# Attention of two units at a time, pairs of heads outermost, and one more weight unit beside it

## The reference

```python
# 1: attention, 2 sequences x 8 heads x 768 positions x 64
scores = q @ k.T / sqrt(64)
keep = (column < 8) | ((row - column >= 0) & (row - column < 96))
scores = where(keep, scores - slope[head] * distance, -1e9)
a = softmax(scores); attn = a @ v                # -> x, 1536 x 512
# 2: soft mixture: 32 slots, 4 for each of 8 experts
logits = x @ phi; d = softmax(logits, over tokens); c = softmax(logits, over slots)
slot_out[e] = relu((d.T @ x)[e] @ w1[e]) @ w2[e]
x = c @ slot_out
# 3: sparse mixture: each token goes to the 2 best of 8 experts
out[token] += weight * (relu(x[token] @ w1[e]) @ w2[e])
```

## Time and profile before

| | |
|---|---|
| median of 3 runs | 392.98 us (391.38 to 393.2) |
| the profiled execution: its own time | 392.51 us |
| the profiled execution: its span | 389.8 us |
| TensorE, VectorE, ScalarE, GpSimd busy | 93%, 49%, 44%, 55% |
| transfers | 88.85 MB, mean 228 GB/s |
| attention, first matmul to the last heads | about 10 to 108 us |
| dispatch and layer 2 | about 108 to 162 us |
| layer 3 | about 162 to 377 us |

### The profile page before, as it was taken

The page is one execution under the profiler, slowest core; times in us unless marked ns, Lnnn a source line. Parts: engine busy times, 40 slices in busy tenths (PEclk is TensorE's granted clock), DMA queues, the critical chain, the costliest instruction groups (busy, mean ns, idle before and its releaser), DMA issues.

```text
span 389.8 us, 8657 instructions
## 1 busy us (share of the span) xinstructions
PE 362.6 (93%) x2892; PEld 251.6 (65%) x2892; DVE 192.7 (49%) x639; ACT 170.4 (44%) x429; POOL 213.3 (55%) x422
## 2 busy tenths in 40 slices
PE   6899999999997999589799999999999999999990
PEld 5566666666564443256577777777777777777770
DVE  2699988888853011068172452623525426254210
ACT  2566777776541110043273453524525336253310
POOL 3568866667811040011446777747766576766741
PEclk9699999999999999889899999999999999999996
DMA  7987999999799999998577899876869762332432
GB/s 161 238 243 224 222 268 298 279 258 374 278 401 347 401 398 387 398 405 330 174 268 170 249 269 250 236 170 145 267 145 209 224 139 34 43 47 32 57 43 38
DMA packets 71976, 88.85 MB, mean 228 GB/s; under 512 B 41616, under 2 KB 42112, under 8 KB 71936
## 3 DMA queue, kind: packets, MB, share of 16 engines
q1 hardware_dynamic: 66448, 79.84, 62.7%
q0 software_dynamic: 5200, 8.49, 15.4%
q10 hardware_dynamic: 288, 0.00, 0.0%
HBM read 77.33 MB, written 10.99 MB: 227 GB/s over the span
## 4 chain that ended last, share of the span: by engine, by line
PE 59%; DVE 16%; issue 15%; DMA 8%; ACT 1%; DVEq 1%; POOL 0%; POOLq 0%; ACTq 0%
PE y_bank L1574 26%; PE y_bank L1577 13%; DMA weight_ring<-in_moe_w 6%; PE h_banks L1563 5%; DVE arena L1031 4%; DVE row_sum L1039 4%; PE bank L1509 3%; PE bank L1261 2%; PE y_bank L1478 2%; DVE row_inv L1053 2%; PE h_banks L1446 2%; PE h_banks L1261 1%; DVE arena L933 1%; DVE arena L1047 1%; DMA counts_i<-in_n_local 1%
## 5 line engine op out<-in xcount | busy, mean ns | idle before, releaser
L1213 DVE SCALAR_TENSOR_TENSOR hT_lo<-h_banks,hT_hi 128x512 fp32r<-128x512 f32 x56 | 38.5, 689 | 110.3 <-ACT hT_hi L866 104.8
L1574 PE MATMUL y_bank<-w_hi,hT_hi 128*128 128x512 f32 x224 | 91.6, 409 | 0.8 <-ACT hT_hi L866 0.8
L1574 PE MATMUL y_bank<-w_lo,hT_hi 128*128 128x512 f32 x224 | 88.2, 394 | 0.0
L866 ACT ACTIVATE hT_hi<-h_banks 128x512 fp32r<-128x512 f32 x56 | 33.4, 597 | 98.8 <-PE y_bank L1577 51.8
L610 POOL TENSOR_TENSOR arena<-arena,row_inv 128x512 f32<-128x512 f32 (+1 forms) x48 | 49.5, 1032 | 29.2 <-DVE row_inv L1053 27.1
L547 POOL TENSOR_TENSOR turn_mark<-turn_mark 128x1 f32<-128x1 f32 x135 | 41.4, 310 | 38.1 <-DMA out_rows<-arena,add_row 12.6
L1577 PE MATMUL y_bank<-w_hi,hT_lo 128*128 128x512 f32 x224 | 59.9, 389 | 0.0
L782 ACT ACTIVATE arena<-arena,neg_max 128x256 f32<-128x256 f32 (+1 forms) x96 | 46.3, 483 | 26.8 <-DVE neg_max L1031 25.8
L705 POOL DMA_INDIRECT out_rows<-arena,add_row x28 | 44.8, 1599 | 14.1 <-issue 13.0
L1574 PEld LDWEIGHTS y_bank<-w_hi,hT_hi 128*128 128x128 f32 x224 | 44.2, 197 | 11.2 <-issue 3.0
L1574 PEld LDWEIGHTS y_bank<-w_lo,hT_hi 128*128 128x128 f32 x224 | 42.8, 191 | 7.9
(11 more groups left out here) (196 smaller groups left out, 494.6 us busy)
## 6 DMA issues: line engine op xcount, KB each, us to landing
weight_ring<-in_moe_w SPq DMA_DIRECT2D x16, 2048.0 KB, 13.2
weight_ring<-in_moe_w SPq DMA_DIRECT2D x22, 1024.0 KB, 5.5
arena<-in_moe_w SPq DMA_DIRECT2D x5, 2048.0 KB, 12.1
arena<-in_q SPq DMA_DIRECT2D x16, 192.0 KB, 5.8
arena<-in_k SPq DMA_DIRECT2D x16, 192.0 KB, 5.4
arena<-in_v SPq DMA_DIRECT2D x8, 384.0 KB, 4.8
out_rows<-zero_row SPq DMA_DIRECT2D x2, 1536.0 KB, 10.4
out_rows<-arena,add_row POOLq DMA_INDIRECT x28
```

The lines of the kernel that those rows point to most:

```text
L1213: vec.scalar_tensor_tensor(hidden_of(hT_lo, half), h_banks[half][:, :, 0:FR], 0.0, hidden_of(hT_hi, half), ALU.max, ALU.subtract).then_inc ...
L1574: mm(y_of(i), hT_hi[:, n, :], w[e % 2][:, n, :], start=(n == 0 and w is w_hi), stop=False)
```

## The change

- TensorE, VectorE and ScalarE run over groups of two units, 24 of them. Group s has the scores of units 2s and 2s+1; head h of both units shares one bank (`score_cols`), so the scores of a group wait until all four logits of the group before are read, and VectorE starts a group only when all its scores are there.
- TensorE's turn is now: the transposes of the probabilities of two units (group s-2), four transposes of q and k (in every group up to the last pair, into banks 0 and 3 in turn, which lets them run one store further ahead), the scores of group s, the heads of group s-2.
- VectorE's turn: four logits, then twice the sum, the reciprocal, and the copy of a unit of group s-1. The sums are of the same group as the logits, and no copy lies between sum and reciprocal any more.
- ScalarE's turn: the store of q and k, the store of heads, then four exponentials.
- Pairs of heads are outermost, so pairs 0, 2, 4 and 6 start new heads: two biases are made in each of pairs 0, 2 and 4, into `bias4`, from operands kept in columns of xT.
- Three transposes of x are issued ahead of the last group's transposes of probabilities; only the fourth one remains behind the product with phi.
- Seven units have a place beside attention and are issued after pairs -1 to 5; no zero rows are. After 42 heads SyncE issues unit 7 and then both halves of the zero rows (3 MB), and after all heads units 8 and 9.

The general path (other counts than those given) is adapted and isn't run here. The rest of the diff moves views of memory.

```diff
-    EARLY = 6
-    DURING = 4
+    EARLY = 7
+    DURING = 3
...
-        v_own[0], v_win[0], qT[0], kT[0] = view(2, QB, HD), view(2, QB - 2, HD), view(S), view(QB, WIN)
-
-        bias8 = view(H, BCOLS)
...
+        for s in range(2):
+            v_own[s], qT[s], kT[s] = view(2, QB, HD), view(S), view(QB, WIN)
+        GENERAL_AT = top[0]
+        v_win = [view(2, QB - 2, HD) for _ in range(2)]
+        bias4 = view(4, BCOLS)
         prob = [view(2, WIN) for _ in range(4)]
         probT = [view(2, 2, P) for _ in range(2)]
...
-        v_win[1], v_own[1], qT[1], kT[1] = view(2, QB - 2, HD), view(2, QB, HD), view(S), view(QB, WIN)
...
-        rel, col, penalty = [view(BCOLS) for _ in range(3)]
+        rel, col = [view(BCOLS) for _ in range(2)]
+        rel_kept, penalty = [xT[:, 0:BCOLS // P, hp, :] for hp in (PAIRS - 1, PAIRS - 2)]
...
-        def score_bank(u, h):
-
-            return bank[1 + (2 * u + h) % 3]
+        GROUPS = UPB * B // 2
+        def score_cols(u, h):
...
+            return bank[1 + h][:, u % 2 * WIN + (P if u % QB == 0 else 0):(u % 2 + 1) * WIN]
+        def qk_bank(n):
+            return bank[3 * (n % 2)]
...
-        ZERO_AFTER = (PAIRS - 1, NPAIR - 4)
+        ZERO_PARTS = 2
...
             def load_v(p):
-                b, hp = divmod(p, PAIRS)
+                hp, b = divmod(p, B)
...
-                if p in UNIT_AFTER:
-                    load_unit(UNIT_AFTER.index(p))
...
-
-                    sp.wait_ge(zeros_made, 1)
-                    part = ZERO_AFTER.index(p)
-                    first, end = [TT * n // len(ZERO_AFTER) for n in (part, part + 1)]
-                    sp.dma_start(out.rearrange("(n p) d -> p n d", p=P)[:, first:end, :],
-                                 zero_row[:].unsqueeze(1).to_broadcast([P, end - first, DM])).then_inc(rows_zeroed, 16)
+                load_unit(p + 1)
...
-                if n == EARLY + 2:
+                if n == EARLY + 1:
+                    sp.wait_ge(zeros_made, 1)
+                    for part in range(ZERO_PARTS):
...
+                        sp.dma_start(out.rearrange("(n p) d -> p n d", p=P)[:, rows, :],
+                                     zero_row[:].unsqueeze(1).to_broadcast([P, TT // ZERO_PARTS, DM])).then_inc(rows_zeroed, 16)
...
                     sp.wait_ge(heads_ready, UPB * B)
...
+                def next_pair(s):
+                    n = s + 3
+                    if n < 3 * NPAIR:
+                        store_qk(n // 3 % 2, n % 3, n, qk_bank(n))
+                for s in range(GROUPS + 3):
+                    if 0 < s < GROUPS:
+                        next_pair(s)
+                    for w in (2 * s - 6, 2 * s - 5):
+                        if w >= 0 and w % HALF == HALF - 1:
+                            store_heads(w // HALF, w + 1)
+                    if s < GROUPS:
+                        for u in (2 * s, 2 * s + 1):
+                            off = P if u % QB == 0 else 0
+                            for h in range(2):
+                                act.wait_ge(logits_ready, 2 * u + h + 1)
+                                own = prob[u % 4][:, h, off:]
+                                last = nc.scalar.activation(own, own, ACT.Exp, bias=neg_max[:, u % 2, h:h + 1], scale=-1.0,
+                                                            accum_out=row_sum[:, u % 4, h:h + 1])
+                            last.then_inc(exps_ready, 1)
+                    if s == 0:
+                        next_pair(s)
...
+                vec.scalar_tensor_tensor(by_block(bias4[:, h % 4, :]), rel_kept, -SLOPES[h] / SCALE, penalty, ALU.mult, ALU.add).then_inc(bias_made, 1)
...
+                    dve.wait_ge(exps_ready, u + 1)
+                    vec.tensor_scalar(row_sum[:, u % 4, :], row_sum[:, u % 4, :], EPS, None, ALU.add).then_inc(sums_ready, 1)
+                    dve.wait_ge(sums_ready, u + 1)
+                    vec.reciprocal(row_inv[:, u % 4, :], row_sum[:, u % 4, :]).then_inc(inv_ready, 1)
+                def store_probT(u):
...
+                for s in range(GROUPS + 1):
+                    p, j = divmod(s, 3)
+                    if s < GROUPS:
+                        if j == 0 and p % B == 0:
+                            dve.wait_ge(bias_made, 2 * (p // B + 1))
+                        dve.wait_ge(scores_ready, s + 1)
+                        if s >= 2:
+                            dve.wait_ge(probT_ready, 2 * s - 2)
...
-                        dve.wait_ge(sums_ready, w + 1)
-                        vec.reciprocal(row_inv[:, w % 4, :], row_sum[:, w % 4, :]).then_inc(inv_ready, 1)
-                    if p < PAIRS - 1 and i in (2, 4):
-                        make_bias(2 * (p + 1) + i // 2 - 1)
+                        for k in range(2):
+                            logits(2 * s + k)
+                    for k in range(2):
+                        if s < GROUPS:
+                            sums(2 * s + k)
+                        if s >= 1:
+                            store_probT(2 * s - 2 + k)
+                    if j and p % B == 0 and p // B + 1 < PAIRS:
+                        make_bias(2 * (p // B + 1) + j - 1)
...
+            def first_x():
+                pe.wait_ge(out_bank_free, HALVES * B)
+                for t in range(3):
+                    transpose_x(t)
...
+                def scores(s):
+                    p, j = divmod(s, 3)
+                    if j == 0:
...
+                        pe.wait_ge(window_ready, 2 * p + 1)
...
+                        pe.wait_ge(window_ready, 2 * p + 2)
+                    if s >= 1:
...
+                        pe.wait_ge(logits_ready, 4 * s)
+                    for u in (2 * s, 2 * s + 1):
...
+                            last = mm(score_cols(u, h), qT[p % 2][own, i * P:(i + 1) * P],
+                                      kT[p % 2][own, i, off:], start=True, stop=True)
                     last.then_inc(scores_ready, 1)
...
+                def transpose_next(s):
+                    n = s + 3
+                    if n < 3 * NPAIR:
+                        p, j = divmod(n, 3)
+                        if j == 0:
+                            pe.wait_ge(qk_loaded[p % 2], QK_DMAS * (p // 2 + 1))
+                        pe.wait_ge(qk_stored, n - 1)
+                        transpose_qk(p % 2, j, n, qk_bank(n))
...
+                for s in range(GROUPS + 2):
+                    if s == GROUPS + 1:
+                        pe.wait_ge(logits_ready, 4 * GROUPS)
+                        first_x()
+                    if s >= 2:
+                        for u in (2 * s - 4, 2 * s - 3):
+                            transpose_probs(u)
+                    if 0 < s < GROUPS:
+                        transpose_next(s)
+                    if s < GROUPS:
+                        scores(s)
+                    if s == 0:
+                        transpose_next(s)
+                    if s >= 2:
+                        for u in (2 * s - 4, 2 * s - 3):
+                            heads(u)
...
-            for t in range(2, 4):
-                transpose_x(t)
+            transpose_x(3)
```

More of the change, by code:

```diff
@@ L469, in _ @@
             load_v(1)
-            UNIT_AFTER = [p for p in range(-1, NPAIR - 2) if p != PAIRS - 1]
-            assert len(UNIT_AFTER) == EARLY
+            assert NPAIR - 1 == EARLY
             for p in range(-1, NPAIR - 2):
@@ L746, in store_heads @@
             def store_heads(hv, done):
[L748 to L749 removed]
+                p, half = divmod(hv, QB // HALF)
+                hp, b = divmod(p, B)
+                token = S * b + half * HALF * P
                 act.wait_ge(heads_ready, done)
[L751 removed]
+                copy(xT[:, token // P:token // P + HALF, hp, :],
                      bank[6 + hv % 2][:, 0:HALF * P].rearrange("p (t n) -> p t n", n=P)).then_inc(out_bank_free, 1)
@@ new lines, in logits @@
+                def logits(u):
+                    hp = u // QB // B
+                    n0, nb = bias_cols(u % QB)
+                    for h in range(2):
+                        vec.tensor_tensor_reduce(
+                            out=prob[u % 4][:, h, WIN - nb:], in0=score_cols(u, h),
+                            in1=bias4[:, hp % 2 * 2 + h, n0:n0 + nb], scale=-SCALE, scalar=3.0e38,
+                            op0=ALU.add, op1=ALU.min, accum_out=neg_max[:, u % 2, h:h + 1]).then_inc(logits_ready, 1)
@@ L1273, in transpose_qk, with transpose_x @@
                 last.then_inc(qk_transposed, 1)
+            def transpose_x(t):
+                if t >= 4:
+                    pe.wait_ge(x_stored_vec if t % 2 else x_stored_act, (t - 4) // 2 + 1)
+                for c in range(DC):
+                    last = transpose(bank[t % 4][:, c * P:(c + 1) * P], xT[:, t, c, :])
+                last.then_inc(x_ready, 1)
+            def first_x():
+                pe.wait_ge(out_bank_free, HALVES * B)
+                for t in range(3):
+                    transpose_x(t)
             pe.wait_ge(consts_made, 1)
```

125 lines of the change are left out of this document (27 added, 98 removed).

## The result

The changed kernel takes 394.5 us (median of 18 executions, 392.4 to 403.4), the kernel before, on the same chip, 391.7 (387.8 to 399.4, 18 executions). The ratio is 1.0083, 95% interval 1.0054 to 1.0112: slower by 0.8%, 3.3 us. Ratios compare only executions outside a slower state that either kernel now and then falls into (up to 403 us here), so they can differ a little from the ratio of the medians. The range of the prediction (388 to 398) holds the median; its likeliest case, no change within 0.5%, did not happen.

The account below looks back on a forecast made before the run. TensorE was taken to bound attention, then transfers released by `part_ready`; VectorE would become attention's bound. `part_ready` 0.3 later takes the profiled 392.5 to 392.8; the median, 0.5 above, gives 393.2, range 388.0 to 398.0.

Parts of the forecast that it names:

- The three rivals in attention: Attention: sum ahead of product, 389.0, nearly all of 0.33; TensorE kinds stay dear, 395.7, 0.17; whole GpSimd hold, 400, 0.05.
- the fourth, by transfers: Transfers: zero rows at two thirds of the rate end the backlog at 126.7, 1.5 longer; chance 0.06.
- no change: Whole kernel: time within 0.5%, 2 us, for itself 391.3 to 395.2; chance 0.39.
- 395.7: Rival in attention: TensorE's kinds stay as dear as now, group 4.05, pair 11.5, 2 more and 0.5; chance 0.17.
- Each bias now costs its whole 0.80 less an overlap of 0.07.: VectorE without slack in attention: six biases in pairs 0, 2 and 4 make these 12.5.
- Pair without bias 11.0: VectorE in attention: groups of 3.2, 3.8 and 4.0 make 11.0 a pair, more than TensorE's 10.8.
- The first logits stay at 11.66: Start of attention: first two biases and first load of q and k as before, so no shift.
- The last pair: End of attention: last heads about 108.75, product with phi at 109.3, 0.3 later than before.
- The 42nd heads at 97.1, the backlog through 2 us ahead of unit 10.: SyncE's transfers: heads 2.4 earlier; 9.4 MB at 404 GB/s end at 122.5 or 123.1, unit 10's first bytes at 125.2.
- the end moves with `part_ready`: Layer 2's transfers: unit 15 lands 36.3 behind `part_ready`, if transfers issued before it are through by then.
- TensorE 3.8 a group: TensorE in attention: 3.8 a group against about 4.0 before, 10.8 a pair, 0.8 less.
- the first rival: Attention: second sum slips ahead of GpSimd's product, TensorE holds the pairs at 10.8, 4.2 less, 389.0; nearly all of 0.33.

Follow-up runs that it names:

- experiments 3: Changed kernel without the additions of 1e-9 to the sums of exponentials: 386.7 us, ratio 0.9851 to the kernel before.
- experiment 4: Changed kernel with two more transposes of probabilities a group on TensorE: ratio 1.0032 to the kernel before.
- 7: Kernel before without the additions of 1e-9 to the sums of exponentials: ratio 0.9972.
- experiment 1: Changed kernel without the six biases VectorE makes inside attention, later heads reusing those of heads 0 and 1: ratio 0.9974 to the kernel before.
- experiment 2: Changed kernel with the two operands of the biases in one contiguous piece of the weight ring's last slot: ratio 1.0057 to the kernel before.
- experiment 5: Changed kernel with both additions to the sums kept, the group's second sum moved behind both copies: 388.9 us, ratio 0.9912 to the kernel before.
- 8: Changed kernel without the additions to the sums, SyncE issuing q and k ahead of the weight unit: 388.3 us, ratio 0.9846 to the kernel before.
- 9: Changed kernel with its twelve first transposes of x back behind the last heads: ratio 1.0078 to the kernel before.
- 11: Changed kernel without additions to the sums, q and k ahead of weight units, biases inside attention by ScalarE: 383.4 us, ratio 0.9785 to the kernel before.
- 12: Changed kernel with ScalarE's biases, q and k ahead of weight units, both additions kept, the second behind both copies: 388.4 us, ratio 0.9867.
- experiment 10: Changed kernel with three useless matrix products ahead of the first scores and four behind them: 395.4 us, ratio 1.0107 to the kernel before.

## What the prediction had right and wrong, step by step

The picture held: VectorE became the bound (experiments 3 and 4 against 7), the second sum is held to the end of GpSimd's product, and nothing is won by what TensorE spares. The three rivals in attention did not happen; the fourth, by transfers, did in part. The sizes missed by 1.7 us at `part_ready`, forecast at 122.8 and measured at 124.5, and the chance of 0.39 for "no change" went with them. That 394.5 nevertheless lies within the 391.3 to 395.2 given for that case is luck: the forecast started from a median of 392.98, and the kernel before then measured 391.7. Of the rivals, 395.7 is the nearest number, but experiment 4 excludes its mechanism.

- **"Each bias now costs its whole 0.80 less an overlap of 0.07."** This is the term that failed. Beside GpSimd a bias takes 0.93 or 1.28 (47.21 above), because it waits for GpSimd's operation and then takes its own 0.67 (rows in the last section). Pairs 2 and 4 took 13.16 and 13.18 where 12.5 was forecast. The pair behind pair 2 gave 0.34 back, so its two biases cost 1.65, those of pair 4 about 2.0; forecast was 1.5. All six held up pair 7 by about 5.4 (experiment 1) where 4.5 was forecast: 0.9 of the 1.7. I had priced them by the row 45.11 0.80, and had looked for GpSimd's hold at the sums alone.
- **Pair without bias 11.0**: 10.84 in pairs 1 and 3, 11.20 and 11.19 in pairs 5 and 6. Groups 3.12 or 3.46, 3.83, 3.90 against 3.2, 3.8, 4.0. Right in size; experiment 1, without biases, has 11.18. The sum of all distances came out 1.26 over the forecast, +1.34 from pairs 2 and 4, +0.39 from pairs 5 and 6, -0.47 from the other three.
- **"The first logits stay at 11.66"**: 12.07, because the operands moved into columns of xT (11.54 with contiguous operands, experiment 2). It cost nothing by itself, since the second group starts at 14.6 with or without it.
- **The last pair**: 16.18 where 16.1 was forecast, 15.68 before.
- **The 42nd heads at 97.1, the backlog through 2 us ahead of unit 10.** They came at 98.9, and by the forecast's own 2 + 23.4 the backlog would end at 124.3, 2.6 ahead of unit 10's first bytes (124.5 + 2.4). Yet no gap was left, which I had named as a sign of being wrong. So the rate failed too. In the stretch in which zero rows were written it was not 375 or 404 (windows of the changed kernel):

```profile
104.00:106.00 2.00, 0.83 (x12) 0.65 (x14) 1.63 (x4) 0.80 (x3) 1.70 (x2) 1.00 0.87 238
106.00:108.00 2.00, 2.00 (x23) 1.83 (x21) 0.00 (x0) 0.00 (x0) 2.00 (x8) 1.00 0.92 324
```

  That is about 1.2 us of transfers lost against 404. From 98 to 124 us 8.8 MB moved (339 GB/s), so of the backlog of 9.4 MB 0.6 MB were left, and it ended near 125.6 or later (an estimate from these rates). The fourth rival's rate, two thirds, came true for these 4 us; its 1.5 at the end did not. In the changed kernel the price is small: unit 15 lands 36.6 behind `part_ready`, not 36.3. But where `part_ready` follows the issue of unit 7 more closely, the backlog and no longer `part_ready` sets the end: with 24.5 to 25.2 us between the two (experiments 3, 5, 8, 9, 11 and 12) unit 15 lands 37.0 to 37.7 behind `part_ready`, with 25.7 (the changed kernel, 2, 4 and 10) 36.1 to 36.6; experiment 1, a slower execution, has 25.7 and 37.2. So "the end moves with `part_ready`" held only just. The 358 GB/s weighed in that step (the Trainium skill, SBUF — State Buffer, Summary: rules for kernel authors) are passed here too, with 418 and 390 in the first two windows above: the trace disagrees with that page again.
- **TensorE 3.8 a group**: about 3.5, from rows with no wait (experiment 4). Heads take 1.03 for two units and not 1.18, scores 1.06 and not 1.12. I had taken distances in a kernel in which each kind stood alone. This did not change the sum, but it made the first rival worth 4.2 in the text; when experiment 5 took most of the hold away, 5.0 came at pair 7 and 6.7 in time.

Of the 3.3 us measured, 2.35 are followed from rows. The other 0.9 is not followed. It is less than single profiles differ by from the last expert on, and the drop of the clock at the start can have a part in it; how often that drop comes to either kernel stays open. The two profiles compared here differ in it: the kernel before was granted 0.50 from 12 to 18 us, the changed one 1.00. What the drop costs the old order is not known, since all three profiles of it have one.

## What to carry to other kernels

When an engine becomes the bound, price its instructions by what they take beside the other engines in the new order, not by the shortest row of the old one; small operations and long ones are held differently. Look for the instruction that waits in the middle of such a chain and move it, before taking work away: the order of two small sums was worth about as much as all six biases (6.7 us of time against 4.3; 5.0 at pair 7 against about 5.4). When a backlog is to be hidden behind a later event, follow it by the bytes that moved and not by the best rate. And when a step speeds one engine, list who gives slack back and who is late next (here q and k behind a 2 MB unit).

## What was not expected of the hardware

- A `tensor_scalar` of 128x2 on VectorE is held by GpSimd's product (0.53 in place of 0.17), a `reciprocal` of 128x2 is not (0.17 in the midst of one), nor are the copies from PSUM (0.69 throughout). The bias, which reads two arrays from SBUF, is held, and holds GpSimd in turn. Pair 2 of the changed kernel, VectorE and then GpSimd:

```profile
42.54 0.93 DVE L948 SCALAR_TENSOR_TENSOR arena<-arena 128x640 f32<-128x640 f32 x1
```

```profile
42.29 0.51 POOL L586 COPY arena<-arena 128x384 f32<-128x384 f32 x1
42.76 1.61 POOL L613 TENSOR_TENSOR arena<-arena,row_inv 128x512 f32<-128x512 f32 x1
...
46.77 1.04 POOL L613 TENSOR_TENSOR arena<-arena,row_inv 128x512 f32<-128x512 f32 x1 [0.30 <-DVE row_inv L1045]
```

  GpSimd's copy ends at 42.80 and the bias 0.67 later; the product from 46.77 ends at 47.81, and the bias that was issued at 47.21 ends 0.68 later (48.49). The product from 42.76 ends 0.90 behind the first bias. Each waits for the whole of the other. The Trainium skill, SBUF — State Buffer, Who interferes with whom, describes such a hold: one exclusive lock, whoever issues first blocks the other, for `tensor_scalar` in a mode that takes both ports and for operations with both inputs in SBUF against a GpSimd operation that reads SBUF. The traces agree with the blocking (which mode the small sum ran in no run here shows); read for the bias and not only for the sum, it would have pointed at the missing term ahead of the run.
- The granted clock between 12 and 14 us was 1.00 in eight profiles of the new order and 0.56 to 0.67 in three, with nearly the same work ahead of it (one of the eight, experiment 10, had the useless products).
